# A gated delta-rule attention with two dense blocks: output products over stacked partitions, right-hand sides and kept halves of two tiles joined

## Chip, cores and metric

One core of one Trainium2 chip. The metric is the device time of one execution in microseconds (us); lower is better.

## The reference, cut to what matters

For 4 batches and 8 heads, 768 tokens, head size 48: with k normalised to length one, a 48 x 48 state per head is read by q (the output) and updated by the delta rule. The result (3072 tokens x 384) then goes through two dense blocks.

```python
for t in range(S):
    kt, vt, bt = (k_n[:, :, t], v[:, :, t], beta[:, :, t, None])
    y[:, :, t] = np.einsum('bhd,bhde->bhe', q[:, :, t], state)
    v_old = np.einsum('bhde,bhd->bhe', state, kt)
    state = state + bt[:, :, :, None] * np.einsum('bhd,bhe->bhde', kt, vt - v_old)
# first block:  ((x @ w1) * (x @ w2)) @ w3 @ w_out
# second block: softmax-weighted units, layer norm, @ w_out
```

## The kernel before

**Chunks.** The recurrence is turned into products over chunks of 64 tokens (`C`). A tile holds one chunk of two batches (`bb` = 0 and 1, on partitions 0 to 63 and 64 to 127); two tiles `g` = 0, 1 (the two pairs of batches) go side by side, and a group `n` holds two such pairs `tt` = 0, 1: 6 groups (`NG`) of 4 tiles (`TPG`). Inside a tile every product is made once per head and batch, 16 small matmuls. Each fp32 matmul leaves two records in the trace, so 16 products read x32.

**One pair of tiles, on TensorE** (`group`, function by function): `k_state` (L1334) takes k times state; VectorE's `right_hand` (L1016) makes v minus that; `apply_inverse` (L1351) multiplies by the inverse of a 32 x 32 triangular block, ScalarE's `keep_u` (L1185) keeps the first half of u; `cross_half` (L1363), `right_hand2` (L1025), `apply_inverse` and `keep_u` again give the second half. `outputs` (L1378 and L1380) makes y as two accumulating products per head and batch, q times state (48 rows) and the masked q k^T (`pt`, 64 rows) times u. `add_state` (L1391) adds k^T u to the state that stays in PSUM, and `keep_state` (L1198) copies it to `st`. Then y is transposed (L1406) and split into high and low halves as input of the first dense block.

**One group ahead.** During the pair `tt` = 0 of group n, `grams` (L1322) makes the products k k^T and q k^T of the four tiles of group n + 1, into one pair of PSUM banks: ScalarE copies the diagonal blocks (`keep_diagonal`, L1164) and the corner (`keep_corner`, L1172), VectorE masks the rest into `pt` (`keep_pt`, L894), and only then the next tile's `grams` may start. From the diagonal blocks VectorE solves the triangular systems of group n + 1 (L900 to L1008: `system_rows`, `coefficients`, `substitute`, `eights_*`, `below_*`, `stationary`) in pieces that are put between its other work. POOL turns two small blocks and scales v.

**Fills.** Between these steps TensorE works on the dense block: `fill` puts one unit `up` (L1422, 18 matmuls of 128 x 256) into each of 8 slots of a pair; unit i waits for VectorE's product (L1044) of unit i - 2. In group 0 there is nothing yet to work on, and the slots take parts of w3 times w_out instead (`w3_wout`, L1435, 128 x 384, 64 parts of which 40 run ahead of group 0 and `FILLS` spreads 24). The order on every engine is written out by hand in `group` of `tensor`, `vector`, `scalar` and `sync`. The state of a tile, `kqs`, holds k and q of a head side by side, on partitions 64 * bb to 64 * bb + 47.

**Opening.** SP's and ScalarE's queues load k and q of group 0, then w3 and w_out. TensorE warms up, makes the first four grams, and waits for w_out.

```python
for bb in range(2):
    rk = slice(64 * bb, 64 * bb + D)
    r = slice(64 * bb, 64 * bb + C)
    if q >= NP:
        pe.matmul(chain[g][r, hc(h)], kqs[rk, par, tile, h, C:P], st[rk, g, hc(h)], start=True, stop=False)
    ins = pe.matmul(chain[g][r, hc(h)], pt[r, par, tile, h, :], uu[r, g, hc(h)], start=q < NP, stop=True)
```

## Time and profile before

| what | value |
|---|---|
| median of 3 runs | 785.2 us (782.42 to 785.26) |
| the profiled execution, whole | 785.01 us |
| its span, first to last instruction | 782.9 us |
| mean granted TensorE clock | 0.993 of full |
| TensorE busy | 758.2 us, 97% of the span |
| VectorE, ScalarE, POOL busy | 58%, 44%, 8% |

A line of the timeline is: start in us, duration in us, engine, line, operation, what it writes and reads, how many, and in brackets the idle time before it with what ended it. Instructions on TensorE overlap, so their rate is read from the starts of neighbouring lines and not from their own durations. All times are on the clock of the span.

### The profile page before, as it was taken

How to read it: one execution, taken by the hardware profiler on the slowest of the kernel's cores; microseconds unless marked ns; L12 is line 12 of the kernel's file. 1: busy time of each engine (PE TensorE's matmuls, PEld its weight loads, DVE VectorE, ACT ScalarE, POOL GpSimd, SP SyncE). 2: the span in 40 equal slices, each digit the busy share in tenths (PEclk: the TensorE clock that was granted, in tenths of full speed). 3: DMA queues.
4: the chain of work that ended last, by engine and by line, in shares of the span. 5: the costliest groups of instructions: out<-in, count | busy, mean ns of one | idle time of the engine just before them, and what ended most of it. 6: DMA issues, size and time to landing. Idle time of an engine off the chain costs nothing.

```text
span 782.9 us, 22421 instructions
## 1 busy us (share of the span) xinstructions
PE 758.2 (97%) x9594; PEld 684.0 (87%) x9594; DVE 457.7 (58%) x782; ACT 347.6 (44%) x750; POOL 64.4 (8%) x96
## 2 busy tenths in 40 slices
PE   7999899999999999999999999999999999999997
PEld 6567799989989998998999888888899999999987
DVE  2955945974794598388522354443366656665663
ACT  5745346235434623634234344444344444445443
POOL 1560200100010010001000000000000000000000
PEclk9999999999999999999999999999999999999999
DMA  9940460342035025103101476540000000000001
GB/s 296 396 103 23 106 163 30 70 110 83 30 83 150 30 69 139 54 30 117 42 30 44 155 242 192 159 147 1 1 21 21 22 22 22 23 23 21 21 20 31
DMA packets 37551, 65.38 MB, mean 84 GB/s; under 512 B 3992, under 2 KB 26648, under 8 KB 36504
## 3 DMA queue, kind: packets, MB, share of 16 engines
q1 hardware_dynamic: 34760, 58.48, 25.3%
q10 hardware_dynamic: 2704, 5.60, 2.3%
q8 instruction: 71, 1.16, 0.7%
q14 instruction: 16, 0.13, 0.1%
HBM read 45.19 MB, written 18.87 MB: 82 GB/s over the span
## 4 chain that ended last, share of the span: by engine, by line
PE 84%; DVE 7%; DMA 3%; ACT 2%; issue 2%; SPq 0%; DVEq 0%
PE ps L1422 24%; PE ps L542 13%; PE ps L506 13%; PE ps L519 12%; PE ps L1322 5%; PE ps L1378 3%; DVE tmp L970 3%; PE ps L531 3%; PE ps L1380 3%; PE ps L1334 3%; DMA vs<-in_vtok 2%; PE ps L1435 2%; PE ps L1391 2%; PE ps L1351 1%; DVE rr L1025 1%
## 5 line engine op out<-in xcount | busy, mean ns | idle before, releaser
L1227 ACT COPY asb<-ps 128x256 f32<-128x256 f32 x96 | 35.8, 373 | 154.3 <-PE ps L1422 153.5
L1044 DVE TENSOR_TENSOR msb<-asb,ps 128x256 f32<-128x256 f32 x96 | 39.9, 415 | 87.3 <-ACT asb L1227 82.1
L542 PE MATMUL ps<-woh,uth 128*128 128x384 f32 x192 | 64.7, 337 | 0.5 <-DVE utl L459 0.5
L542 PE MATMUL ps<-woh,utl 128*128 128x384 f32 x192 | 64.5, 336 | 0.0
L542 PE MATMUL ps<-wol,uth 128*128 128x384 f32 x192 | 64.3, 335 | 0.0
L1422 PE MATMUL ps<-xh,w1h 128*128 128x256 f32 x288 | 57.3, 308 | 6.6 <-DVE msb L1044 6.6
L894 DVE TENSOR_TENSOR pt<-ps,mask 128x512 f32<-128x512 f32 x24 | 16.6, 690 | 77.2 <-ACT a L1172 77.2
L459 DVE TENSOR_TENSOR utl<-ps,uth 128x512 fp32r<-128x512 f32 x48 | 31.1, 687 | 47.9 <-ACT uth L349 47.9
L335 ACT ACTIVATE e<-ps,stats 128x1024 f32<-128x1024 f32 x24 | 26.8, 1117 | 67.6 <-DVE stats L425 67.6
L506 PE MATMUL ps<-mh,w34h 128*128 128x512 f32 x144 | 56.0, 389 | 0.0
L506 PE MATMUL ps<-ml,w34h 128*128 128x512 f32 x144 | 56.0, 389 | 0.0
L506 PE MATMUL ps<-mh,w34l 128*128 128x512 f32 x144 | 56.0, 389 | 0.0
L1185 ACT COPY uu<-ps 32x384 f32<-32x384 f32 x96 | 45.2, 471 | 14.4 <-PE ps L1351 13.2
L1422 PE MATMUL ps<-xh,w2h 128*128 128x256 f32 x288 | 50.8, 286 | 0.0
L1422 PE MATMUL ps<-xl,w2h 128*128 128x256 f32 x288 | 50.8, 286 | 0.0
L1422 PEld LDWEIGHTS ps<-xh,w1h 128*128 128x128 f32 x288 | 40.7, 191 | 11.5 <-DVE msb L1044 7.4
L1422 PE MATMUL ps<-xh,w1l 128*128 128x256 f32 x288 | 50.6, 285 | 0.0
L1422 PE MATMUL ps<-xh,w2l 128*128 128x256 f32 x288 | 50.6, 285 | 0.0
L1422 PE MATMUL ps<-xl,w1h 128*128 128x256 f32 x288 | 50.1, 282 | 0.0
L1322 PE MATMUL ps<-kqs 48*64 48x128 f32 x768 | 46.9, 273 | 2.7 <-DVE pt L894 1.2
L1322 PEld LDWEIGHTS ps<-kqs 48*64 48x64 f32 x768 | 42.3, 134 | 7.1 <-issue 6.6
L431 DVE SCALAR_TENSOR_TENSOR mfirst<-ps,e 128x1024 f32<-128x1024 f32 x24 | 29.4, 1225 | 31.8 <-ACT e L335 31.8
(155 smaller groups left out, 1744.5 us busy)
## 6 DMA issues: line engine op xcount, KB each, us to landing
m_dram<-msb SPq DMA_DIRECT2D x42, 256.0 KB, 2.1
mrest<-m_dram SPq DMA_DIRECT2D x36, 256.0 KB, 5.9
kqs<-in_kq SPq DMA_DIRECT2D x20, 384.0 KB, 7.4
vs<-in_vtok SPq DMA_DIRECT2D x6, 768.0 KB, 11.0
ks<-in_ktok SPq DMA_DIRECT2D x5, 768.0 KB, 7.0
mfirst<-m_dram SPq DMA_DIRECT2D x12, 256.0 KB, 5.6
out<-wst SPq DMA_DIRECT2D x12, 192.0 KB
out<-wst SPq DMA_DIRECT2D x48, 48.0 KB, 1.5
```

The source lines that it names most:

```text
L335: act.activation(e[:, :], hb[s], ACT.Exp, bias=nmax[:, s:s + 1], accum_out=es[:, s:s + 1]).then_inc(expd, 1)
L431: dve.scalar_tensor_tensor(out=ubuf[:, s, :], in0=hb[s], scalar=1.0, in1=e[:, :], op0=ALU.mult, op1=ALU.mult, accum_out=us[:, s:s + 1]).th ...
L459: dve.tensor_tensor(utl[:, j, :, :], tb[j].rearrange("p (k c) -> p k c", c=P), uth[:, j, :, :].bitcast(F32), ALU.subtract).then_inc(ut_low, 1)
L506: ins = pe.matmul(hbank[par][k], w[:, f, k * P:(k + 1) * P], mm[:, u, f % UF, :, :].rearrange("p t c -> p (t c)"), start=(f == 0 and j == ...
L519: ins = pe.matmul(hb[slot % 2][:, c * 512:(c + 1) * 512], xx[:, slot, k, :], w[:, k, c * 512:(c + 1) * 512], start=(j == 0 and k == 0), st ...
L531: ins = pe.transpose(tb[j][:, k * P:(k + 1) * P], ubuf[:, s, c:c + P], ident[:, :])
L542: ins = pe.matmul(ob[s], xx[:, j, k, :], w[:, 4 * j + k, :], start=(j == 0 and k == 0 and p == 0), stop=(j == 1 and k == 3 and p == 2))
L1044: dve.tensor_tensor(msb[:, f // 2 % 2, f % 2, :], asb[:, f % 2, :], bbank[f % 2], ALU.mult).then_inc(product, 1)
L1185: ins = act.copy(uu[rows, g, :], chain[g][rows, :])
L1227: act.copy(asb[:, f % 2, :], abank[f % 2]).then_inc(a_kept, 1)
L1322: ins = pe.matmul(gbank[64 * bb:64 * bb + C, h, :], kqs[r, par, tile, h, 0:C], kqs[r, par, tile, h, :], start=True, stop=True)
L1422: ins = pe.matmul(bank, w[:, k, cols], xx[:, par, k, :], start=(j == 0 and k == 0), stop=(j == 2 and k == KD - 1))
```

## The change

The state moves onto the other half of the partitions: of batch `bb` it now stands on partitions 64 * (1 - bb), below or above that batch's u, in one buffer `us`; q stands in `kqs` in the same way beside the masked q k^T, which VectorE now writes into `kqs` as well. So `outputs` makes one product per head and batch over 112 or 128 partitions in place of two. `k_state` and `grams` read rows of the other half than they write. The mask of a tile takes two instructions of 64 partitions. `right_hand` and `right_hand2` take one instruction of 128 x 768 for both tiles, `keep_u` two of 64 x 768. In the opening, k is loaded ahead of q and has its own grams (64 columns), those with q come after three of the w3 products; w_out moves to ScalarE's queue; diagonals are copied ahead of corners; `FILLS` and `WARM` change, and in group 0 the first gram of group 1 follows `apply_inverse`, and `eights_first` and `eights_products` follow `right_hand`.

```diff
-        kqs = buf("kqs", [P, 2, TPG, H, P])
+        kqs = buf("kqs", [P, 2, TPG, 3, H, C])
...
-        pt = buf("pt", [P, 2, TPG, H, C])
...
-        uu = buf("uu", [P, NP, DM])
+        us = buf("us", [P, NP, 2, DM])
         ysb = buf("ysb", [P, NP, DM])
-        st = buf("st", [112, NP, DM])
...
+        both = ps[:, 0:NP, 0:DM]
         gbank = ps[:, 2:4, :].rearrange("p b (h c) -> p (b h) c", c=P)
-        first_gbank = [ps[:, b:b + 2, :].rearrange("p b (h c) -> p (b h) c", c=P) for b in (4, 6, 0, 2)]
+        first_a = [ps[:, b, :].rearrange("p (h c) -> p h c", c=C) for b in (0, 1, 6, 7)]
+        first_p = [ps[:, b, :].rearrange("p (h c) -> p h c", c=C) for b in (2, 3, 6, 7)]
...
-        FILLS = {(0, 0): 3, (0, 1): 3, (0, 2): 3, (0, 3): 3, (0, 4): 3, (0, 5): 3, (0, 6): 2, (0, 7): 2, (1, 0): 2}
+        FILLS = {(0, 0): 6, (0, 1): 4, (0, 2): 3, (0, 3): 3, (0, 4): 2, (0, 5): 2, (0, 6): 1, (0, 7): 1, (1, 0): 2}
         FIRST_W34 = KF - 3
-        WARM = 9
+        WARM = 6
...
+        def state_rows(bb):
+            return slice(64 * (1 - bb), 64 * (1 - bb) + D)
+
+        def loaded_rows(bb):
+            return slice(64 * (1 - bb), 64 * (1 - bb) + (64 if bb else D))
+
+        def u_rows(bb):
+            return slice(64 * bb, 64 * bb + C)
+
+        STACK = (slice(0, 64 + D), slice(0, P))
...
-                    sp.dma_start(kqs[64 * bb:64 * bb + D, n % 2, 2 * tt:2 * tt + 2, :, :],
-                                 kq[n, bb, :, tt]).then_inc(kq_in[n % 2][tt], 16)
+                    r = loaded_rows(bb)
+                    for part in range(2):
+                        sp.dma_start(kqs[r, n % 2, 2 * tt:2 * tt + 2, part * (1 + bb), :, :],
+                                     kq[n, bb, 0:r.stop - r.start, tt, :, part]).then_inc(kq_in[n % 2][tt], 16)
...
-            for tile in range(TPG):
-                sp.dma_start(kqs[0:D, 0, tile:tile + 1, :, :],
-                             kq[0, 0, :, tile // 2, tile % 2:tile % 2 + 1]).then_inc(kq_first[tile], 16)
+            def load_first(part, tt, arrived):
+                sp.dma_start(kqs[loaded_rows(0), 0, 2 * tt:2 * tt + 2, part, :, :],
+                             kq[0, 0, 0:D, tt, :, part]).then_inc(arrived[tt], 16)
+
+            for tt in range(2):
+                load_first(0, tt, k_first)
             load_w3(0)
-            sp.dma_start(wos[0], wo1[:, 0:4, :]).then_inc(wo1_in[0], 16)
             load_w3(1)
+            for tt in range(2):
+                load_first(1, tt, q_first)
+            load_w3(2)
             load_v(0)
-            for f in range(2, 5):
-                load_w3(f)
-            for j in range(2 * KF):
+            load_w3(3)
+            for j in range(KF):
                 load_w(j)
+            load_w3(4)
+            sp.wait_ge(w34_done, 2)
+            load_kq(1, 0)
             load_w3(5)
-            load_k(1)
+            for j in range(KF, 2 * KF):
+                load_w(j)
+            sp.wait_ge(w34_done, 4)
+            load_kq(1, 1)
             for f in range(6, KF):
                 load_w3(f)
-            sp.wait_ge(w34_done, 2)
-            load_kq(1, 0)
-            sp.wait_ge(w34_done, 4)
-            load_kq(1, 1)
+            load_k(1)
             sp.wait_ge(w34_done, KF)
             load_v(1)
             for n in range(1, NG):
...
+            const(pool.memset(us[HB:C, :, 1, :], 0.0))
...
-            def keep_pt(n, par, tile, gbank=gbank):
-                i = TPG * n + tile
-                dve.wait_ge(gram_kept, i + 1)
-                dve.tensor_tensor(pt[:, par, tile, :, :], gbank[:, :, C:P],
-                                  mask[:, tile % NP, :].unsqueeze(1).to_broadcast([P, H, C]), ALU.mult).then_inc(pt_made, 1)
+            def masked(par, tile, bank):
+                for bb in range(2):
+                    r = u_rows(bb)
+                    ins = dve.tensor_tensor(kqs[r, par, tile, 1 + bb, :, :], bank[r],
+                                            mask[r, tile % NP, :].unsqueeze(1).to_broadcast([C, H, C]), ALU.mult)
+                ins.then_inc(pt_made, 1)
+
+            def keep_first_pt(tile):
+                dve.wait_ge(p_gram, tile + 1)
+                masked(0, tile, first_p[tile])
+
+            def keep_pt(n, par, tile):
+                dve.wait_ge(gram_kept, TPG * n + tile + 1)
+                masked(par, tile, gbank[:, :, C:P])
...
-            def right_hand(n, par, tt, g):
-                q = TPG * n + NP * tt + g
-                dve.wait_ge(ks_done, q + 1 - NP)
-                dve.wait_ge(v_scaled, n + 1)
-                tile = NP * tt + g
-                dve.tensor_tensor(rr[:, g, :], vs[:, par, tile * DM:(tile + 1) * DM], chain[g],
-                                  ALU.subtract).then_inc(rhs, 1)
-
-            def right_hand2(n, tt, g):
-                q = TPG * n + NP * tt + g
-                dve.wait_ge(cross, q + 1)
-                for bb in range(2):
-                    rows = half_rows(bb, g, 1)
-                    before = vs[rows, 0, g * DM:(g + 1) * DM] if q < NP else rr[rows, g, :]
-                    ins = dve.tensor_tensor(rr[rows, g, :], before, chain[g][rows, :], ALU.subtract)
-                ins.then_inc(rhs2, 1)
+            def of_both(par, tt):
+                return vs[:, par, NP * tt * DM:NP * (tt + 1) * DM].rearrange("p (g n) -> p g n", n=DM)
+
+            def right_hand(n, par, tt):
+                dve.wait_ge(ks_done, TPG * n + NP * tt)
+                if n == 0:
+                    dve.wait_ge(v_first, 2)
+                else:
+                    dve.wait_ge(v_scaled, n)
+                dve.tensor_tensor(rr[:, :, :], of_both(par, tt), both, ALU.subtract).then_inc(rhs, NP)
+
+            def right_hand2(n, tt):
+
+                q = TPG * n + NP * tt
+                dve.wait_ge(cross, q + NP)
+                given = of_both(0, 0) if q < NP else rr[:, :, :]
+                dve.tensor_tensor(rr[:, :, :], given, both, ALU.subtract).then_inc(rhs2, NP)
...
-                    right_hand(n, par, 0, 0)
-                    right_hand(n, par, 0, 1)
+                    right_hand(n, par, 0)
                 product_of(0, 0)
...
+                right_hand(n, par, 1)
+                if n == 0:
+                    eights_first(n + 1)
+                    eights_products(n + 1)
...
-            dve.wait_ge(consts, 11)
-            for tile in range(3):
-                keep_pt(0, 0, tile, first_gbank[tile])
+            dve.wait_ge(consts, 12)
             system_rows(0)
...
-            keep_pt(0, 0, 3, first_gbank[3])
+            for tile in range(TPG):
+                keep_first_pt(tile)
...
-            def keep_u(q, g, half, done, kept):
-                act.wait_ge(done, q + 1)
+            def keep_u(q, half, done, kept):
+
+                act.wait_ge(done, q + NP)
                 if q == 0 and half == 0:
                     act.wait_ge(w_low, 2 * NP)
-                for bb in range(2):
-                    rows = half_rows(bb, g, half)
-                    ins = act.copy(uu[rows, g, :], chain[g][rows, :])
-                ins.then_inc(kept, 1)
+                    for g in range(NP):
+                        for bb in range(2):
+                            rows = half_rows(bb, g, half)
+                            ins = act.copy(us[rows, g, bb, :], chain[g][rows, :])
+                else:
+                    for bb in range(2):
+                        ins = act.copy(us[u_rows(bb), :, bb, :], both[u_rows(bb)])
+                ins.then_inc(kept, NP)
...
-                    rows = slice(64 * bb, 64 * bb + D)
-                    ins = act.copy(st[rows, g, :], sbank[g][rows, :])
+                    rows = state_rows(bb)
+                    ins = act.copy(us[rows, g, bb, :], sbank[g][rows, :])
...
                     a_of(0)
-                    if early:
+                    if early and n > 0:
                         keep_gram(n + 1, 0)
-                    keep_u(q, 0, 0, u1_done, u1_kept)
-                    keep_u(q + 1, 1, 0, u1_done, u1_kept)
+                    keep_u(q, 0, u1_done, u1_kept)
+                    if early and n == 0:
+                        keep_gram(n + 1, 0)
...
+            def load_first(part, tt, arrived):
+                act.dma_start(kqs[loaded_rows(1), 0, 2 * tt:2 * tt + 2, 2 * part, :, :],
+                              kq[0, 1, :, tt, :, part]).then_inc(arrived[tt], 16)
+
+            for tt in range(2):
+                load_first(0, tt, k_first)
+            act.dma_start(wos[0], wo1[:, 0:4, :]).then_inc(wo1_in[0], 16)
             act.dma_start(bet[:, :, :], beta).then_inc(beta_in, 16)
             act.dma_start(wos[1], wo1[:, 4:8, :]).then_inc(wo1_in[1], 16)
+            for tt in range(2):
+                load_first(1, tt, q_first)
             act.dma_start(ks[:, 0, :], ktok[0]).then_inc(k_in[0], 16)
             act.preload_act_table(ACT.Sqrt)
-            keep_gram(0, 0, first_gbank[0])
-            keep_gram(0, 1, first_gbank[1])
-            keep_gram(0, 2, first_gbank[2])
-            keep_gram(0, 3, first_gbank[3])
+            for tile in range(TPG):
+                keep_diagonal(0, tile, first_a[tile])
+            keep_corner(0, 0, first_a[0])
+            keep_corner(0, 1, first_a[1])
             roots(0)
-            scale_first_v()
-            for f in range(FIRST_W34):
-                for j in range(4 * f - 4, min(4 * f, 2 * KF)):
-                    if j >= 0:
-                        high_w(j)
+            keep_corner(0, 2, first_a[2])
+            keep_corner(0, 3, first_a[3])
+            for f in range(2):
+                keep_w34(f)
+                scale_first_v(f)
+            for f in range(2, FIRST_W34):
+                for j in range(4 * (f - 2), min(4 * (f - 1), KF)):
+                    high_w(j)
...
+            def first_grams(part, tile, bank, done):
+                for h in range(H):
+                    for bb in range(2):
+                        r = state_rows(bb)
+                        ins = pe.matmul(bank[u_rows(bb), h, :], kqs[r, 0, tile, 0, h, :],
+                                        kqs[r, 0, tile, part * (1 + bb), h, :], start=True, stop=True)
+                ins.then_inc(done, 1)
...
-                        r = slice(64 * bb, 64 * bb + D)
-                        ins = pe.matmul(gbank[64 * bb:64 * bb + C, h, :], kqs[r, par, tile, h, 0:C],
-                                        kqs[r, par, tile, h, :], start=True, stop=True)
+                        r = state_rows(bb)
+                        ins = pe.matmul(gbank[u_rows(bb), h, :], kqs[r, par, tile, 0, h, :],
+                                        kqs[r, par, tile, 0:2 + bb:1 + bb, h, :], start=True, stop=True)
...
-                        rk = slice(64 * bb, 64 * bb + D)
-                        r = slice(64 * bb, 64 * bb + C)
-                        if q >= NP:
-                            pe.matmul(chain[g][r, hc(h)], kqs[rk, par, tile, h, C:P], st[rk, g, hc(h)],
-                                      start=True, stop=False)
-                        ins = pe.matmul(chain[g][r, hc(h)], pt[r, par, tile, h, :], uu[r, g, hc(h)],
-                                        start=q < NP, stop=True)
+                        r = STACK[bb] if q >= NP else u_rows(bb)
+                        ins = pe.matmul(chain[g][u_rows(bb), hc(h)], kqs[r, par, tile, 1 + bb, h, :],
+                                        us[r, g, bb, hc(h)], start=True, stop=True)
                 ins.then_inc(y_done, 1)
...
-                    if early:
+                    if early and n > 0:
                         grams(n + 1, 0)
                     if tt == 0:
                         pe.wait_ge(inverse, n + 1)
                     apply_inverse(n, par, tt, 0, rhs, u1_done)
+                    if early and n == 0:
+                        grams(n + 1, 0)
...
-                grams(0, tile, first_gbank[tile])
-            pe.wait_ge(gram_kept, 1)
-            pe.wait_ge(pt_made, 1)
+                pe.wait_ge(k_first[tile // 2], 32)
+                first_grams(0, tile, first_a[tile], gram)
             for half in range(2):
                 for f in range(2):
                     w3_wout(f, range(KF // 2 * half, KF // 2 * (half + 1)))
             for f in range(2, FIRST_W34):
                 w3_wout(f, range(KF))
-            pe.wait_ge(gram_kept, 3)
-            pe.wait_ge(pt_made, 3)
+                if f == 2:
+                    for tile in range(TPG):
+                        pe.wait_ge(q_first[tile // 2], 32)
+                        if tile >= 2:
+                            pe.wait_ge(gram_kept, tile + 1)
+                        first_grams(1, tile, first_p[tile], p_gram)
+            pe.wait_ge(gram_kept, TPG)
...
-        return split(a).transpose(3, 1, 7, 4, 0, 2, 5, 6)
+        return split(a).transpose(3, 1, 7, 4, 0, 2, 5, 6).reshape(NG, 2, D, 2, NP, H * C)
...
-        "kq": np.stack([columns(k), columns(q)], axis=6).reshape(NG, 2, D, 2, NP, H, P),
+        "kq": np.pad(np.stack([columns(k), columns(q)], axis=5), [(0, 0), (0, 0), (0, 64 - D)] + [(0, 0)] * 4),
```

How the rows stand on TensorE at the outputs of the second pair of group 0 (a row of `order` is line, operation, out<-in, shape, count; `xh`, `xl`, `w2l` belong to `up`). Before:

```order
L1422 MATMUL ps<-xh,w2h 128x256 x3
L1422 MATMUL ps<-xl,w2h 128x256 x3
L1422 MATMUL ps<-xh,w2l 128x256 x3
L1378 MATMUL ps<-st,kqs 64x48
L1380 MATMUL ps<-uu,pt 64x48
...
L1391 MATMUL ps<-uu,ks 48x48 x16
```

After the change:

```order
L1472 MATMUL ps<-xh,w2l 128x256 x3
L1430 MATMUL ps<-us,kqs 64x48 x16
L1441 MATMUL ps<-us,ks 48x48 x16
L1430 MATMUL ps<-us,kqs 64x48 x16
L1441 MATMUL ps<-us,ks 48x48 x16
L1472 MATMUL ps<-xh,w1h 128x256 x3
```

The alternating rows of L1378 and L1380, 16 of each a tile, have become 16 of L1430.

On VectorE, from the first pair of group 1 on (L1044 is the product of a unit, L900 the start of the next solve). Before:

```order
L1016 TENSOR_TENSOR rr<-vs,ps 128x384 x2
L1044 TENSOR_TENSOR msb<-asb,ps 128x256
L894 TENSOR_TENSOR pt<-ps,mask 128x512
L1044 TENSOR_TENSOR msb<-asb,ps 128x256
L894 TENSOR_TENSOR pt<-ps,mask 128x512
L1025 TENSOR_TENSOR rr<-rr,ps 32x384 x4
```

After:

```order
L1053 TENSOR_TENSOR rr<-vs,ps 128x768
L1078 TENSOR_TENSOR msb<-asb,ps 128x256
L918 TENSOR_TENSOR kqs<-ps,mask 64x512 x2
L1078 TENSOR_TENSOR msb<-asb,ps 128x256
L918 TENSOR_TENSOR kqs<-ps,mask 64x512 x2
L1060 TENSOR_TENSOR rr<-rr,ps 128x768
```

The right-hand sides have shrunk from 2 and 4 instructions to 1 each, the mask has grown from 1 to 2.

On TensorE's opening after the change (L1360 are the first grams, k's above and q's below; before, 64 products of 64x128 stood in the first place and none in the second):

```order
L1540 MATMUL ps<-ident 128x128 x6
L1360 MATMUL ps<-kqs 64x64 x64
L1485 MATMUL ps<-vs,kqs 128x384 x8
L1485 MATMUL ps<-mfirst,kqs 128x384 x8
L1485 MATMUL ps<-vs,kqs 128x384 x4
L1485 MATMUL ps<-mfirst,kqs 128x384 x4
L1360 MATMUL ps<-kqs 64x64 x64
```

The products with q have moved behind the first 24 parts of w3 times w_out.

## Rows read from the trace of the kernel before

**Rows 1.** The page: share of the chain that ended last.
```profile
PE 84%; DVE 7%; DMA 3%; ACT 2%; issue 2%; SPq 0%; DVEq 0%
```

**Rows 2.** Timeline, TensorE, outputs of the second pair of group 2.
```profile
229.94 0.52 PE L1422 MATMUL ps<-xh,w2l 128*128 128x256 f32 x3
230.39 0.33 PE L1378 MATMUL ps<-st,kqs 48*64 48x48 f32 x4
...
232.29 0.92 PE L1391 MATMUL ps<-uu,ks 64*48 64x48 f32 x32
233.01 0.32 PE L1378 MATMUL ps<-st,kqs 48*64 48x48 f32 x4
...
234.88 0.92 PE L1391 MATMUL ps<-uu,ks 64*48 64x48 f32 x32
```

**Rows 3.** Timeline, TensorE, outputs of the first pair, which has no state.
```profile
67.58 1.14 PE L1380 MATMUL ps<-uu,pt 64*64 64x48 f32 x32
68.55 0.89 PE L1391 MATMUL ps<-uu,ks 64*48 64x48 f32 x32
```

**Rows 4.** Chain of waits: start, us, what.
```profile
29.97 17.65 PE ps L1435 x54
...
159.45 3.50 PE ps L1422 x18
168.67 2.35 PE ps L1422 x18
```

**Rows 5.** Timeline, TensorE, transposes between two units.
```profile
207.83 0.82 PE L1406 MATMUL ps<-ident,ysb 128*128 128x128 f32 x6
208.40 0.60 PE L1422 MATMUL ps<-xh,w1h 128*128 128x256 f32 x3
```

**Rows 6.** Timeline, one turn of the gram banks: TensorE, ScalarE, VectorE.
```profile
247.39 1.96 PE L1322 MATMUL ps<-kqs 48*64 48x128 f32 x32
...
252.64 1.96 PE L1322 MATMUL ps<-kqs 48*64 48x128 f32 x32
...
249.40 1.49 ACT L1164 COPY gd<-ps 32x256 f32<-32x256 f32 x4 [1.53 <-PE ps L1322]
250.91 0.74 ACT L1172 COPY a<-ps 32x256 f32<-32x256 f32 x2
...
251.68 0.69 DVE L894 TENSOR_TENSOR pt<-ps,mask 128x512 f32<-128x512 f32 x1 [3.36 <-ACT a L1172]
```

**Rows 7.** Timeline, last gram of a group to the last third of its second pair.
```profile
196.00 1.96 PE L1322 MATMUL ps<-kqs 48*64 48x128 f32 x32
217.23 0.88 PE L1351 MATMUL ps<-rr,ti 32*32 32x48 f32 x64
228.05 0.62 PE L1422 MATMUL ps<-xh,w1h 128*128 128x256 f32 x3 [0.16 <-DVE msb L1044]
...
214.37 1.18 DVE L1016 TENSOR_TENSOR rr<-vs,ps 128x384 f32<-128x384 f32 x2
...
222.97 2.26 DVE L1025 TENSOR_TENSOR rr<-rr,ps 32x384 f32<-32x384 f32 x4
```

**Rows 8.** Costliest groups: a VectorE subtraction of 128 x 768.
```profile
L218 DVE TENSOR_TENSOR w34l<-h,w34h 128x768 fp32r<-128x768 f32 x3 | 2.9, 959 | 1.1 <-ACT w34h L210 1.1
```

**Rows 9.** Opening: a DMA issue (line, count, KB, us to landing) and the timeline.
```profile
vs<-in_wo SPq DMA_DIRECT2D x1, 768.0 KB, 13.8
...
17.07 7.05 PE L1435 MATMUL ps<-vs,kqs 128*128 128x384 f32 x16 [3.57 <-DMA vs<-in_wo]
...
63.55 1.96 PE L1322 MATMUL ps<-kqs 48*64 48x128 f32 x32 [0.33 <-DVE pt L894]
...
82.65 0.88 PE L1351 MATMUL ps<-rr,ti 32*32 32x48 f32 x64 [2.71 <-DVE rr L1016]
...
16.67 1.93 DVE L900 STREAM_TRANSPOSE amat<-gd 128x1024 f32<-128x1024 f32 x1 [0.82 <-ACT gd L1164]
...
44.93 2.10 DVE L1008 STREAM_TRANSPOSE ti<-xt 128x1024 f32<-128x1024 f32 x1
```

63 lines of the change are left out of this document (29 added, 34 removed).

## The prediction

> **What bounds it now.** The chain of waits comes first: TensorE is 84% of what ended last, VectorE 7% [rows 1]. So a microsecond of TensorE's work is a microsecond of the kernel, except where TensorE stands and waits for VectorE. The timeline of the attention part then shows three things. One: the outputs of a tile take 230.39 to 232.29 and 233.01 to 234.88, 1.90 and 1.87 us for 64 records [rows 2]. Two: the grams turn in a ring. A gram starts at 247.39, the next at 252.64, 5.25 us later, and between them lie its own 1.96, ScalarE's copies to 251.65, and VectorE's mask from 251.68 to 252.37 [rows 6]: each begins when the one before ends, so the ring sets the pace and TensorE's other work of that turn fits inside it. Three: in the second pair TensorE is ready for a unit at about 226.5 and starts it at 228.05, after VectorE [rows 7].
>
> **How fast a product of 48 columns can go.** Full-array fp32 products of 384 columns run at 17.65 / 54 = 327 ns a record [rows 4], so 0.85 ns a column and 41 ns for 48 columns. The masked products alone (64 rows, 64 weight columns, 48 moving columns, `bb` alternating) need 0.97 us for 32 records, 30 ns each [rows 3], and the pair of products 1.87 / 64 = 29 ns [rows 2]. That is under 41, so the two halves of the array, with different rows and different columns, work at once. The state update has 48 weight columns and takes 0.72 / 32 = 22.5 ns [rows 2]: the rate goes with the weight columns, 0.45 ns each, so loading sets it.
>
> **Term 1, the outputs.** 22 of 24 tiles (all but the first pair) drop from 64 records to 32. The unknown is a record's price. The two products of a head now use all the rows and only differ in columns; no row of this trace has that. Bounds: 29 ns if they still overlap; 41 ns and a few for the start, 43 to 51, if they stream one after the other; 41 plus a load of 64 columns at 0.45, 70 ns, if the load is not hidden either; and 95 ns, the step of the 128-column transposes, (208.40 - 207.83) / 6 [rows 5], as the far end. I take 29, since its row is the same stationary and moving size on the same engine and only the row group differs. Then a tile saves 0.94 us, a pair 1.87. Against that, outputs and state update no longer share an array shape. Going from a unit to the products costs 0.09 us (229.94 + 3 x 0.12 = 230.30, start at 230.39) [rows 2]; three more such changes a pair cost 0.27. Net 1.6 us a pair.
>
> **Term 2, the ring.** The mask becomes two instructions of 64 partitions with the same 512 elements each. A VectorE instruction's time goes with elements per partition (384 take 0.57 to 0.59 in a row of four or two [rows 7], 512 take 0.69 alone [rows 6], of which some 0.07 overlaps the next), so the second adds about 0.62. It lies in the ring: three turns in each of five groups, 9.3 us if nothing gives. This is a real loss that the change brings with it: after 247.39 the last gram comes 17.6 us later in place of 15.7. k_state, the state update and the grams reading one half and writing the other keep their sizes: nothing.
>
> **Term 3, the right-hand sides.** `right_hand` becomes one instruction of 768: 0.96 [rows 8] for 1.18; `right_hand2` one of 0.96 for 2.26 [rows 7], 1.3 less. From the last gram (196.00) to VectorE's right-hand side (215.55) are 19.5 us of nearly unbroken VectorE work, and TensorE reaches its use at 217.23, 1.7 later [rows 7]. Now VectorE needs 19.5 + 0.6 - 0.2 = 19.9, TensorE 21.2 - 1.6 = 19.6: VectorE is just ahead as the bound, and takes back 0.5 of the first pair's gain. From there to 228.05 the old way is 12.5; minus 1.3 for `right_hand2` and minus 1.0 that VectorE idled for ScalarE's copy of a unit (which is now long there) gives 10.2. Last gram to that unit: 32.05 before, 30.2 now, 1.85 less.
>
> **Groups 1 to 4**: +1.87 (ring) - 1.85 - 1.6 (outputs of the second pair) = -1.6 each, -6.4. In group 1 the wait was followed by a unit of 3.50 us in place of 2.35 [rows 4], which no other group shows; I put it down to the clock falling in the wait, and with a shorter wait it should go: -1.2. **Group 5** has no ring and no solve: 2 x 1.6 = -3.2. ScalarE's `keep_u` loses a little; it was hidden behind the units and stays hidden. Doubled DMA issues of k and q are on SP's queue, which has microseconds between them.
>
> **Opening and group 0.** TensorE waited until 17.07 for w_out, issued at 3.12 and landed 13.8 later behind 4 x 192 KB of k and q and 512 KB of w3 on one of two queues [rows 9]: 2048 KB in some 15 us, 137 KB/us a queue. Now it follows 512 KB on the other queue: 1280 KB, so near 11. The 46 parts ahead of the inverse take 46 x 0.65 = 29.9, the four grams of q 4.2, waits 0.7: 45.8. VectorE's solve began at 16.67 and its last step ended at 47.0 [rows 9]. The k grams are half as wide and the 16 diagonal copies (4 x 1.5 us) come first: start near 13.3, end 43.6. So the inverse is applied near 46, but the four masks of group 0 (2 x 0.65 each) now stand behind the solve, to 48.8, and the second gram of group 1 waits for them and for its own: 52.3. With two turns of 5.86 the last gram starts at 64.0, against 63.55 [rows 9]. Then 4 us of solve steps have moved behind the right-hand side, which TensorE had waited 2.71 for [rows 9]: it comes 3.0 earlier, and the moved 4 us delay the later part of that pair by about as much. With its outputs, group 0 ends 0.5 to 2.5 earlier; I take -1.2.
>
> **Sum**: -1.2 - 6.4 - 1.2 - 3.2 = -12.0 on the profiled 785.0, so 773.0. The median of the runs is 0.2 above the profiled one, which changes nothing. A change of 0.5% (about 4 us) is what a measurement of this kernel can tell from none.
>
> **Rivals.**
> *The columns stream in turn.* Two products that use the same rows might share what feeds the rows, so they go one after the other at 43 to 51 ns, 47 in the middle. For it: nothing in the trace shows overlap with common rows. Against it: nothing but likeness. A tile then takes 1.50 and saves 0.37; a pair nets 0.5 in place of 1.6, over 11 pairs 12 us less gain, of which VectorE's bound in four first pairs returns 2 to 3. Result 773 + 9.5 = 782.
> *The weights are not hidden* (the other side). `bb` alternates row groups now, and the load for one half can run while the other multiplies; with all rows in use by both there is no other half. Price 70 ns, 2.2 us a tile: 0.35 slower than before, and 0.27 for the shapes, about +1.0 a pair against -1.6. Over 11 pairs 28 us worse than my sum; the first pairs of groups 1 to 4 get back 0.5 each, and waits for VectorE shrink by some 4 more: 773 + 22 = 795. It decides from about 47 to 49 ns a record on, where the sum passes zero. Against it: full-array records show a load of 128 columns hidden behind a stream at 327 ns for 384 columns, so a load of the same rows can be hidden, though there the stream is long.
> The Trainium skill (TensorE: Matmul & The Clock Gate, Part 3, the mechanism) says that a weight load overlaps matmuls in flight only when the row group differs. By that rule the change would come out at this rival; the full-array rows speak against taking it literally, and the page itself excepts the background weight buffer. The Trainium skill (TensorEngine Tiling, key properties) says on the other side that tiles of 128 x 64 are two and load and multiply independently, which is my forecast; no run here shows it yet.
> *The opening does not come earlier.* If both queues share the bandwidth otherwise and TensorE starts near 14 to 17, its extra 6 us ahead of the inverse (grams of q, 3 more parts) show: group 0 ends 4 to 7 later, 773 + 6 = 779.
>
> **Chances and range.** Forecast 0.58 (767 to 778, nearly all over 0.5% faster, 0.56 and 0.02); late opening 0.10 (0.07 faster, 0.03 same); columns in turn 0.18, 778 to 787 (0.06 faster, 0.11 same, 0.01 slower); weights not hidden 0.14, 787 to 820, slower. Faster 0.69, same 0.16, slower 0.15. The range takes the first three: 766 to 787.
>
> **What would show it.** Right: 32 records of L1430 start within 0.93 to 1.0 us a tile, with `add_state` rows unchanged at 0.72 and gaps near 0.1 around them; the grams of a group 5.8 to 5.9 apart; the wait before the unit after the second `apply_inverse` under 0.8 us; TensorE's first w3 product near 11. A step of 1.4 to 1.6 us a tile is the first rival, 2.2 or more the second. The forecast is wrong in its base if the ring still turns in 5.25, or if the masks' two halves overlap.

## The result and the profile after

The changed kernel takes 773.6 us (median of 4 runs, 771.74 to 774.38) against 785.05 us (4 runs, 782.42 to 785.26), a ratio of 0.9858 with a 95% interval of 0.9831 to 0.9886: 11.45 us faster, where 12.0 were forecast. The profiled execution has a span of 772.7 us, 10.2 less than the one before. Of the page after, the share of the chain that ended last, and three groups of instructions (busy us, mean ns, idle us before them and what ended it):

```profile
PE 80%; DVE 9%; ACT 6%; issue 4%; DMA 2%; DVEq 0%
...
L918 DVE TENSOR_TENSOR kqs<-ps,mask 64x512 f32<-64x512 f32 x48 | 33.0, 687 | 73.3 <-ACT a L1204 72.8
...
L1472 PE MATMUL ps<-xh,w1h 128*128 128x256 f32 x288 | 57.4, 308 | 6.2 <-DVE msb L1078 6.2
...
L1376 PE MATMUL ps<-kqs 48*64 48x128 f32 x640 | 39.3, 272 | 13.3 <-DVE kqs L918 13.3
```

TensorE is less of the chain than in [rows 1], VectorE and ScalarE more. The last line is the ring: TensorE now waits 13.3 us for masks of 687 ns each. Timeline after, TensorE, from the second `apply_inverse` of the second pair of group 2 over its outputs (they answer to [rows 2] and [rows 7]):

```profile
226.23 0.88 PE L1405 MATMUL ps<-rr,ti 32*32 32x48 f32 x64
227.05 0.63 PE L1472 MATMUL ps<-xh,w1h 128*128 128x256 f32 x3
...
229.39 1.14 PE L1430 MATMUL ps<-us,kqs 112*64 112x48 f32 x32
230.46 0.92 PE L1441 MATMUL ps<-us,ks 64*48 64x48 f32 x32
231.31 1.14 PE L1430 MATMUL ps<-us,kqs 112*64 112x48 f32 x32
232.38 0.92 PE L1441 MATMUL ps<-us,ks 64*48 64x48 f32 x32
233.23 0.62 PE L1472 MATMUL ps<-xh,w1h 128*128 128x256 f32 x3
```

A tile's outputs take 1.07 us from start to start, 33.4 ns a record, in place of 1.90. The unit after `apply_inverse` starts without the wait that [rows 7] has. One turn of the ring after, answering to [rows 6]:

```profile
244.88 1.97 PE L1376 MATMUL ps<-kqs 48*64 48x128 f32 x32
246.89 1.49 ACT L1196 COPY gd<-ps 32x256 f32<-32x256 f32 x4 [1.53 <-PE ps L1376]
248.40 0.74 ACT L1204 COPY a<-ps 32x256 f32<-32x256 f32 x2
249.17 1.39 DVE L918 TENSOR_TENSOR kqs<-ps,mask 64x512 f32<-64x512 f32 x2 [3.36 <-ACT a L1204]
...
250.82 1.96 PE L1376 MATMUL ps<-kqs 48*64 48x128 f32 x32 [0.82 <-DVE kqs L918]
```

5.94 us in place of 5.25: the mask's two halves do not overlap, and the difference is the second one. The opening and group 0 after, answering to [rows 9]:

```profile
6.91 7.09 PE L1360 MATMUL ps<-kqs 48*64 48x64 f32 x128 [2.24 <-DMA kqs<-in_kq]
13.94 1.01 PE L1485 MATMUL ps<-vs,kqs 128*128 128x384 f32 x1
...
49.56 0.88 PE L1405 MATMUL ps<-vs,ti 32*32 32x48 f32 x64
50.37 1.96 PE L1376 MATMUL ps<-kqs 48*64 48x128 f32 x32
...
68.23 1.96 PE L1376 MATMUL ps<-kqs 48*64 48x128 f32 x32 [1.02 <-DVE kqs L918]
...
15.65 1.93 DVE L933 STREAM_TRANSPOSE amat<-gd 128x1024 f32<-128x1024 f32 x1 [15.65 <-ACT gd L1196]
```

Here the last gram is 4.7 us later than before, not 0.5. Where the time went, by marks that both traces have (us from start to start; the grams of a group are those that it makes for the next):

| stretch | before | after | difference | forecast |
|---|---|---|---|---|
| start to the first gram in group 1 | 111.28 | 113.64 | +2.4 | -1.2 |
| to the first gram in group 2 | 68.98 | 65.51 | -3.5 | -2.8 |
| to that in group 3 | 67.13 | 65.73 | -1.4 | -1.6 |
| to that in group 4 | 67.13 | 65.53 | -1.6 | -1.6 |
| to group 5's first `apply_inverse` | 67.14 | 65.94 | -1.2 | -1.6 |
| to the first L506, the next stage | 75.80 | 70.88 | -4.9 | -3.2 |
| to the end of the span | 325.44 | 325.47 | 0.0 | 0 |

The sum of the differences is the span's, -10.2. About 1.5 us of the -4.9 in the last stretch but one was not forecast: before, TensorE waits 1.79 us for VectorE ahead of the last six units, and 0.8 us after it has gone on its records slow down. Over the 4 us shown the mean is 0.58, and from 444 to 447 it is 0.50, the 1.2 GHz level. The kernel before at this place: the wait, three records at the low clock (0.84 us where the others take 0.52), the busy time in 4 us (us and count of PE, PEld, DVE, ACT, POOL, then the granted clock), and the chain of waits before and after:

```profile
442.92 0.62 PE L1422 MATMUL ps<-xh,w1h 128*128 128x256 f32 x3 [1.79 <-DVE msb L1044]
...
444.44 0.84 PE L1422 MATMUL ps<-xh,w2h 128*128 128x256 f32 x3
```

```profile
443.00:447.00 4.00, 4.00 (x22) 4.00 (x23) 2.20 (x3) 0.41 (x2) 0.00 (x0) 0.58 0.17 66
```
```profile
442.92 14.70 PE ps L1422 x108
```
```profile
434.17 13.22 PE ps L1472 x108
```

The wait after is 1.36 us, and the clock stays at 1.00. The slow unit of group 1 in the kernel before [rows 4] looks the same: TensorE waits 1.80 us for VectorE until 159.45, and the granted clock is 0.50 from 161 to 163. A third such stretch of the kernel before is its opening: after the wait for w_out until 17.07 the mean granted clock is 0.60 from 18 to 21. The kernel after has none of the three. The mean clock of its four runs is 0.999 to 1.000, against 0.992 to 0.996 in the 11 runs of before that stand beside the first experiments.

### The profile page after: what moved, and what is told of

It is laid out like the page before. It is cut to its first block, busy times and chain, and to the rows that moved or that the text cites. A ratio compares the mean times of both kernels' runs of the same rounds, so it can differ in the third digit from the quotient of the medians.

```text
span 772.7 us, 21207 instructions
## 1 busy us (share of the span) xinstructions
PE 741.6 (96%) x9012; PEld 664.5 (86%) x9012; DVE 451.2 (58%) x759; ACT 339.5 (44%) x704; POOL 66.6 (9%) x97
## 4 chain that ended last, share of the span: by engine, by line
PE 80%; DVE 9%; ACT 6%; issue 4%; DMA 2%; DVEq 0%
PE ps L1472 19%; PE ps L542 13%; PE ps L506 13%; PE ps L519 12%; PE ps L1376 5%; PE ps L1485 4%; ACT gd L1196 3%; PE ps L1388 3%; PE ps L531 3%; DVE kqs L918 2%; PE ps L1430 2%; ACT a L1204 2%; PE ps L1441 2%; PE ps L1360 1%; PE ps L1405 1%
## 5 line engine op out<-in xcount | busy, mean ns | idle before, releaser
L918 DVE TENSOR_TENSOR kqs<-ps,mask 64x512 f32<-64x512 f32 x48 | 33.0, 687 | 73.3 <-ACT a L1204 72.8
L506 PE MATMUL ps<-mh,w34h 128*128 128x512 f32 x144 | 56.0, 389 | 0.0
L506 PE MATMUL ps<-ml,w34h 128*128 128x512 f32 x144 | 56.0, 389 | 0.0
L506 PE MATMUL ps<-mh,w34l 128*128 128x512 f32 x144 | 56.0, 389 | 0.0
L1376 PE MATMUL ps<-kqs 48*64 48x128 f32 x640 | 39.3, 272 | 13.3 <-DVE kqs L918 13.3
L1196 ACT COPY gd<-ps 32x256 f32<-32x256 f32 x96 | 34.8, 363 | 35.2 <-PE ps L1376 32.2
L1376 PEld LDWEIGHTS ps<-kqs 48*64 48x64 f32 x640 | 34.9, 133 | 17.0 <-issue 16.4
## 6 DMA issues: line engine op xcount, KB each, us to landing
vs<-in_vtok SPq DMA_DIRECT2D x6, 768.0 KB, 10.2
```

What stands on the lines that cost most here:

```text
L506: ins = pe.matmul(hbank[par][k], w[:, f, k * P:(k + 1) * P], mm[:, u, f % UF, :, :].rearrange("p t c -> p (t c)"), start=(f == 0 and j == ...
L918: ins = dve.tensor_tensor(kqs[r, par, tile, 1 + bb, :, :], bank[r], mask[r, tile % NP, :].unsqueeze(1).to_broadcast([C, H, C]), ALU.mult)
L1196: ins = act.copy(gd[rows, tile * H:(tile + 1) * H, :], gbank[rows, :, HB * half:HB * (half + 1)])
L1376: ins = pe.matmul(gbank[u_rows(bb), h, :], kqs[r, par, tile, 0, h, :], kqs[r, par, tile, 0:2 + bb:1 + bb, h, :], start=True, stop=True)
```

## The experiments

**Whose alternation makes the products overlap.** After, with the loops of `outputs` exchanged, so that 8 products for one column half follow each other.

```diff
-                for h in range(H):
-                    for bb in range(2):
+                for bb in range(2):
+                    for h in range(H):
```

> The change with one edit: in the outputs all 8 products of one batch (112 rows, columns 0 to 63) come first, then all 8 of the other (128 rows, columns 64 to 127), in place of by turns. Theory (products on common rows but different columns overlap when they alternate): nothing is left to overlap, a record goes from 33 ns to 41 ns (48 columns at 0.85) and more, 45 to 60, so a tile goes from 1.07 us to 1.45 to 1.9 and the kernel gains 7 to 15 us on 773.6: 781 to 789. Rival (they never overlap and the rate is set by the weight load alone): a record stays at 33 ns and the time at 773 to 775.

Measured: 786.07 us, 1.0035 of before (1.0018 to 1.0051). Timeline of its TensorE:

```profile
231.80 1.87 PE L1430 MATMUL ps<-us,kqs 112*64 112x48 f32 x32
233.60 0.92 PE L1441 MATMUL ps<-us,ks 64*48 64x48 f32 x32
```

The same 32 records need 1.80 us, 56 ns each against 33.4. So the overlap comes from alternating between the two column halves, and without it the whole gain is gone (+12.5 us).

**The price of a product, by doubling it.** After, each stacked product issued twice in a row.

```diff
-                        ins = pe.matmul(chain[g][u_rows(bb), hc(h)], ...
+                        for again in range(2 if q >= NP else 1):
+                            ins = pe.matmul(chain[g][u_rows(bb), hc(h)], ...
```

> The change with each stacked output product issued twice in a row (the second overwrites the first). Theory (TensorE is the bound and a stacked record costs 33 ns): 32 records more in 22 tiles at 33 ns are 1.07 us a tile, 23.5 us, of which the first pairs of groups 1 to 4 give back up to 1 us each because VectorE is ahead there: +19 to +24, 793 to 797. If the same column half twice in a row cannot overlap, a record costs 41 ns or more and the sum is +30 or more. Rival (the outputs are hidden): under +10.

Measured: 794.45 us, 1.0133 (1.0103 to 1.0162), +20.8 against after.

```profile
207.59 2.11 PE L1431 MATMUL ps<-us,kqs 112*64 112x48 f32 x64
209.62 0.92 PE L1442 MATMUL ps<-us,ks 64*48 64x48 f32 x32
```

64 records take 2.03 us, 31.7 ns each; the 32 added ones take 0.96 us a tile, 30 ns each, and 20.8 us over 22 tiles give the same 30. So two neighbours may share a column half as long as the next two take the other. Undoing the stacking itself, two accumulating products in the new layout, was not tried.

**The right-hand sides alone.** Before, with `right_hand` and `right_hand2` joined as in the change.

```diff
-                right_hand2(n, 1, 0)
-                right_hand2(n, 1, 1)
+                right_hand2(n, 1)
...
+                dve.tensor_tensor(rr[:, :, :], given, both, ALU.subtract).then_inc(rhs2, NP)
```

> The kernel before with only the right-hand sides joined (one instruction of 128x768 for both tiles, twice a pair); outputs, masks, copies and opening as before. Theory: right_hand2 ends 1.3 us earlier, the wait of TensorE ahead of the unit after the second apply_inverse (1.4 to 1.9 us in groups 1 to 4) shrinks by 1.3, and the slow unit in group 1 goes: -5 to -7 us, 778 to 780. Rival (VectorE is late there for the contended subtraction and not for right_hand2, or the clock fell for another reason): -2 us or less, 783 to 785.

Measured: 777.47 us, 0.9927 (0.9902 to 0.9952), -7.0 against the 784.49 of before measured with it. So 7 us are to be had with the outputs left as they were, about as much as the split mask costs in the next run. Not all of it is shorter waiting: the granted clock stays at 1.00 both in group 1 and in the last six units, which is worth some 1.2 and 1.5 us.

```profile
436.10 13.21 PE ps L1417 x108
```

Ahead of these six units TensorE waits 1.86 us, longer than the 1.79 of the kernel before, and still they run at full speed. So the length of the wait does not by itself decide whether the clock falls.

**The split mask alone.** Before, with the mask in two instructions of 64 partitions.

```diff
+                for bb in range(2):
+                    r = slice(64 * bb, 64 * bb + C)
+                    ins = dve.tensor_tensor(pt[r, par, tile, :, :], gbank[r, :, C:P], ...
```

> The kernel before with only the mask in two instructions of 64 partitions instead of one of 128. Theory (the mask lies in the ring of grams, copies and mask): each of 15 turns goes from 5.25 us to 5.87, +9.3 us, and VectorE's later work adds up to 0.6 in groups 1 to 4, so 794 to 797. Rival (two halves of the partitions overlap on VectorE, or the ring has slack): within 2 us of 785.

Measured: 791.13 us, 1.0097 (1.0059 to 1.0136): +6.6, less than expected, though the ring turns in 5.94 as expected (grams at 184.57 and 190.52). From the first gram for a group to that for the next it has 252.26 to 319.96, 67.70 us, only 0.57 over before, and from the last gram (270.10) to that mark 49.86 where before has 263.12 to 314.52, 51.40. Something gives back 1.5 us behind the ring. VectorE and POOL at that place, first before, then with the split mask:

```profile
217.49 2.78 POOL L856 TENSOR_TENSOR vs<-vs,nrm 128x1536 f32<-128x1536 f32 x1
218.08 3.28 DVE L970 TENSOR_TENSOR tmp<-amat,xt 128x1024 f32<-128x1024 f32 x1
```
```profile
224.48 1.22 DVE L973 TENSOR_TENSOR tmp<-amat,xt 128x1024 f32<-128x1024 f32 x1
224.56 3.76 POOL L856 TENSOR_TENSOR vs<-vs,nrm 128x1536 f32<-128x1536 f32 x1
```

Before, POOL's scaling of v starts first and VectorE's product of the solve, started 0.59 us later, takes 3.28 us; with the split mask VectorE is 0.08 ahead and takes 1.22, and POOL pays with 3.76 in place of 2.78. The next experiment tests this.

**POOL's scaling out of VectorE's way.** Before, with one wait more.

```diff
                 pool.wait_ge(coef, GCOEF * (n + 1))
+                pool.wait_ge(solve, GSOLVE * n + MERGED8 + 1)
```

> The kernel before with one more wait in POOL's scaling of v (L856): it starts only when VectorE's first wide product of the solve (L970, 128 x 1024) is done. Nothing is left out. In the traces so far L970 takes 3.28 us where POOL's scaling starts 0.59 us ahead of it (217.49 and 218.08, before) and 3.72 us where it starts 0.12 ahead (joined_rhs_alone), but 1.22 us where it starts 0.08 behind (split_mask_alone, batch_outer) and 1.65 in the kernel after (219.27 and 218.74); POOL's own instruction takes 2.78 us when first and 3.75 to 3.79 when second. Theory (the one that starts second pays, and VectorE is what TensorE waits for in the second pair of each group of before): L970 at 1.22, 2.06 us less in each of groups 1 to 4; TensorE's wait there of 1.5 us goes, and one that costs a slow clock behind it in group 1 and ahead of the last six units; last Gram product of a group to the first of the next 51.40 -> 49.8 (that of split_mask_alone is 49.86); in all 777 to 779, so -6 to -8. Rival (VectorE's product is long for a reason of its own, or the collision moves on to L979 or L1025 behind it): L970 or the next instruction longer by 2 us, total 784.7 within 1.5.

Measured: 777.93 us, 0.9921 (0.9898 to 0.9945), -6.7 against 784.6.

```profile
215.85 2.77 POOL L857 TENSOR_TENSOR vs<-vs,nrm 128x1536 f32<-128x1536 f32 x1 [2.03 <-DVE tmp L971]
...
214.36 1.22 DVE L971 TENSOR_TENSOR tmp<-amat,xt 128x1024 f32<-128x1024 f32 x1
215.61 1.22 DVE L980 TENSOR_REDUCE gd<-tmp 128x128 f32<-128x1024 f32 x1
```

The product takes 1.22, the reduction beside POOL's scaling is not stretched, and from the last gram to the next group's first are 49.87 us (257.88 to 307.75). One added wait brings more than half of what the whole change brings. It and the joined right-hand sides shorten the same wait of TensorE; both together were not run on the kernel before, and need not add up.

**The mask released by bank.** After, tiles 0 to 2 masked in four instructions of 64 x 256, heads 0 to 3 first; the next grams of heads 0 to 3 start when their PSUM bank is free.

```diff
+                for part in range(2):
+                    hs = slice(H // 2 * part, H // 2 * (part + 1))
+                    for bb in range(2):
...
+                    ins.then_inc(pt_made if part else pt_low, 1)
```

> The change with the mask of the first three tiles of a group split by PSUM bank as well (four instructions of 64 x 256, heads 0 to 3 of both batches first), and the next grams of heads 0 to 3 released after the first bank, those of heads 4 to 7 after the second. Theory (the mask is in the ring, 5.94 us a turn): the first two instructions take about 0.8 us in place of 1.3 and the second bank's mask runs under the first 8 products, so a turn goes to 5.3 to 5.5 and 15 turns give 6.5 to 9.5 us; VectorE pays 0.3 us more a tile, hidden: 764 to 768. Rival (the next thing behind the ring, ScalarE's copies or VectorE's products, takes it over): 771 to 774.

Measured: 765.82 us, 0.977 (0.9737 to 0.9804), -7.8 against after.

```profile
185.76 1.96 PE L1393 MATMUL ps<-kqs 48*64 48x128 f32 x32 [0.28 <-DVE kqs L936]
...
190.04 1.75 DVE L936 TENSOR_TENSOR kqs<-ps,mask 64x256 f32<-64x256 f32 x4 [2.34 <-ACT a L1215]
191.16 1.96 PE L1393 MATMUL ps<-kqs 48*64 48x128 f32 x32 [0.28 <-DVE kqs L936]
```

The mask itself grew to 1.75 us, but TensorE starts before it ends: 5.40 us a turn, 0.54 less, 15 turns, 8.1 us. The ring's time is the kernel's.

**Outputs of both tiles in one go**, then the state of both.

```diff
                     outputs(n, par, tt, 0)
-                    add_state(n, par, tt, 0)
                     outputs(n, par, tt, 1)
+                    add_state(n, par, tt, 0)
```

> The change with both tiles' outputs first and both state updates after them, so two changes of array shape fewer a pair (unit, out, out, add, add, unit). Theory (a change of shape costs about 0.13 us: add_state takes 0.85 from start to start where it took 0.72): 11 pairs x 0.26 = -2.9, 770 to 772. Rival (the surplus is in the records themselves, or the later keep_state delays k_state): 773 to 775, with 32 records still at 1.07.

Measured: 770.98 us, 0.9836 (0.9799 to 0.9873), -2.6 against after, less than the scatter of four runs can settle by itself (the two intervals overlap). The trace settles it:

```profile
227.95 2.07 PE L1430 MATMUL ps<-us,kqs 112*64 112x48 f32 x64
...
231.53 0.62 PE L1472 MATMUL ps<-xh,w1h 128*128 128x256 f32 x3
```

A pair takes 3.58 us (227.95 to 231.53) in place of 3.84, with two changes between the two kinds of product fewer: each costs about 0.13 us, and 11 pairs give 2.9.

**Both of these**, the mask released by bank and the outputs together, in one kernel.

> bank_gate and outputs_together in one kernel. If their gains are on TensorE's path and independent they add: 761 to 766. If one hides the other, no better than the better of the two.

Measured: 764.29 us, 0.9753 (0.9721 to 0.9785): 20.4 us under before and 9.3 under the change, where the two gains alone add up to 10.4.

**The state's half left out.** After, with products over the 64 rows of u alone: q times state is not computed.

```diff
-                        r = STACK[bb] if q >= NP else u_rows(bb)
+                        r = u_rows(bb)
```

> The change with the state half left out of the outputs: only the 64 rows of masked q k^T times u, one product per head and batch in the 64x64 shape (the q times state part of y is not computed). Theory (a stacked record costs no more than a 64-row one, and the shape changes cost the rest): 32 records take 0.93 us as in the first pair, add_state 0.72, so a pair loses 4 x 0.13: 11 x 0.54 = -6, 767 to 769. Rival (the 112 to 128 rows themselves cost): outputs fall to 0.93 while add_state stays at 0.85.

Measured: 768.79 us, 0.981 (0.9778 to 0.9843), -4.8 against after, with runs from 765.88 to 772.37. Its TensorE:

```profile
225.66 0.96 PE L1430 MATMUL ps<-us,kqs 64*64 64x48 f32 x26
226.41 0.25 PE L1441 MATMUL ps<-us,ks 64*48 64x48 f32 x2
...
228.60 0.62 PE L1472 MATMUL ps<-xh,w1h 128*128 128x256 f32 x3
```

29 ns a record as in [rows 3], and records of the state update stand between those of the outputs: a pair takes 2.94 us (225.66 to 228.60), 0.90 less than after and less than the 3.3 that was expected. So the gain is not one of cheaper records alone: part of it is that the two kinds of product mix, which they do not with full rows. Of the 0.90 us only the second pair's counts: from 175.61 to 240.25, 64.64 us a group against 65.6. In the first pair the gain is lost again: from the last gram to the second pair's outputs are 32.23 us in both kernels (193.43 to 225.66, and 197.16 to 229.39). VectorE is the bound there, as the forecast had it.

**The opening's clock.** After, with 11 opening products in place of 6.

> The kernel after with 11 opening products of the identity in place of 6, so that TensorE doesn't wait 2.24 us for the first k before the first Gram products. Nothing is left out. In the kernel after those products take 1.7 us a tile (7.09 us for four) and four copies of ScalarE follow at this pace, so that VectorE's system starts at 15.65. Theory (the opening is paced by the slow k products): with no wait ahead of them the products run at up to twice the rate, about 1.0 us a tile, ScalarE's copies (1.49 us each) become the bound, the system starts at 13.8 to 14.6, the w_out product starts when its first weights have landed, about 12.6 instead of 13.9, the first inverse is applied at 48.3 instead of 49.6; total 772.4 (771.5 to 773.5), so -1.2 against the kernel after. Rival (TensorE's 36 us of products in the opening are paced by their data and by each other, and the clock of the first Gram products is not set by the wait): products of 1.7 us a tile as now, first inverse at 49.6, total 773.6, no change.

Measured: 773.23 us, 0.988 (0.9829 to 0.993), no difference from after that can be told.

```profile
6.73 2.17 PE L1360 MATMUL ps<-kqs 48*64 48x64 f32 x64
9.31 2.08 PE L1360 MATMUL ps<-kqs 48*64 48x64 f32 x64 [0.40 <-DMA kqs<-in_kq]
12.76 5.40 PE L1485 MATMUL ps<-vs,kqs 128*128 128x384 f32 x16 [1.36 <-DMA vs<-in_wo]
```

The k grams do run at 34 ns a record in place of 55, and the inverse is applied at 47.68 in place of 49.56; the span is 1.1 shorter (771.6), inside the scatter of runs. Now TensorE waits for w_out until 12.76, so 11 was never to be had. The expectation put the slow grams down to the wait ahead of them; the next run speaks against that.

**The old shares of the w_out product.** After, with the old `FILLS`.

> The kernel after with the pieces of the w_out product shared out over group 0's positions as in the kernel before (3, 3, 3, 3, 3, 3, 2, 2 in the first pair in place of 6, 4, 3, 3, 2, 2, 1, 1). Nothing is left out. Theory (in group 0 TensorE waits 1.25, 1.02 and 1.02 us for VectorE's masks between the four Gram products, and pieces ahead of a Gram product stand in those waits, pieces behind the last one do not): four pieces move behind the last Gram product, each 0.36 us a weight tile and two or three of these a piece, so the end of group 0 comes 1 to 3 us later and the total is 774.6 to 776.6. Rival (behind the last Gram product TensorE waits 0.65, 0.81 and 0.34 us for ScalarE and VectorE, which take up what moves there): 773.6, within 0.5.

Measured: 772.62 us, 0.9849 (0.9818 to 0.988): the rival, nothing lost. The new shares bring nothing.

```profile
5.47 7.19 PE L1360 MATMUL ps<-kqs 48*64 48x64 f32 x128 [0.80 <-DMA kqs<-in_kq]
```

Here k came at 5.47 rather than 6.91. TensorE waited 0.80 us for it in place of 2.24, and the grams took 56 ns a record all the same, so the length of that wait is not what slows them. The inverse was applied at 45.52; three shares fewer ahead of it explain 2.0 of the 4.0 us. The rest is scatter: in `batch_outer`, `outputs_doubled`, `outputs_together`, `half_rows` and `bank_gate`, which open just as the kernel after does, the inverse is applied at 46.87 to 48.75, and 49.56 in the kernel after is the latest of all.

**The fastest kernel with the longer opening.**

> The fastest kernel so far (mask released bank by bank, outputs of both tiles in one go, state added for both behind; 764.3) with 11 opening products in place of 6. Nothing is left out. If the wait for the first k costs what the theory on it says, 763.1 (762 to 764.3); by its rival 764.3. Either way the gains of the two earlier edits should stand.

Measured: 763.38 us, 0.9747 (0.9708 to 0.9786), 0.9 under `both_of_these`, which 4 runs each cannot tell from none.

## Why the forecast held, step by step

- **Outputs (term 1): right.** 29 ns a record were taken, 33.4 measured; the changes of shape were put at 0.27 a pair, and beside the dearer record 0.13 shows (the first state update, 0.85 for 0.72). A pair fell from 5.34 to 3.84, 1.50 against 1.6. The rival with columns in turn (43 to 51) and the one with weights not hidden (70) would have shown 1.4 to 2.2 us a tile against the 1.07 measured. `batch_outer` shows how near they were: 56 ns if only the order of the loops is another, past the forecast's own break-even of 47 to 49, and that kernel is indeed 0.35% slower than before. By the rule that the Trainium skill (TensorE: Matmul & The Clock Gate, Part 3) gives, that a weight load overlaps only matmuls of another row group, the two orders should be equally slow, since all these products use rows of every group; the runs disagree, 33.4 against 56 ns. What the Trainium skill (TensorEngine Tiling, key properties) says of column tiles that load and multiply independently agrees with them.
- **The ring (term 2): right in mechanism, a little small.** 5.87 a turn were forecast, 5.94 to 6.14 measured; from first to last gram 18.0 in group 2 where 17.6 were said.
- **Right-hand sides (term 3): right in size, incomplete in cause.** Last gram to unit took 29.89 (197.16 to 227.05) where 30.2 were said and 32.05 was before. VectorE's two instructions are 0.95 each, as [rows 8] promised. But L970's 3.28 us stood in the old trace beside the POOL row that stretched it, and the forecast took VectorE's work there as fixed. After, VectorE starts 0.53 ahead of that POOL instruction and needs 1.65. VectorE's last product before that unit ends at 225.50, 1.55 us early, so in the changed kernel this gift of 1.6 lies in slack (worked out from these rows, not run).
- **Slow clock: half seen.** The unit of 3.50 us in group 1 is gone (group 1 gave 3.5, forecast 2.8). That the last six units lose as much in the same way (14.70 for 13.22) was not seen, and gave 1.5 more. Nor is the mechanism settled: the forecast expected the clock to stay up because the wait is shorter, but in `joined_rhs_alone` it stays up behind a longer one (1.86 us). The low clock is in nearly every run of the kernel before (mean 0.993) and hardly shows in the four after (0.999 to 1.000); what decides it stays open.
- **Opening and group 0: wrong.** +2.4 us in place of -1.2. The step that failed is the start of the w_out product "near 11": its first weights, landed 10.3 us after their issue at 2.26, are there at 12.6, and the k grams held TensorE until 13.94, as k came 2.24 us after the warm-up's end and the grams then took 55 ns a record. Of the 3.6 us by which the inverse is late (49.56 for 46) this is 2.9; the last gram comes at 68.23 for 64.0. The rival "the opening does not come earlier" was right as to the opening, and too dear: behind the last gram 2.3 of the 4.7 us come back (63.55 to 111.28 before, 68.23 to 113.64 after), 1.5 of it from the outputs. The moved solve steps bring little: TensorE's wait of 2.71 us is down to 0.34, but waits of 1.55 and 0.92 us for VectorE follow in the same pair. The 46 was missed in every execution with this opening (46.87 at the best), but part of the +2.4 is the profiled execution's own bad luck. And the inverse is no earlier than before (49.56 for 49.72) although the w_out product starts 3.1 us earlier and the low clock of the old opening is gone: the grams of q and three more shares now stand ahead of it. An estimate of what the rebuilt opening does: `joined_rhs_alone`, with the old one, has its first gram of group 1 at 110.03; three longer turns add 2.1 and the outputs of one pair take off 1.5, so 110.6. With the new opening it is 113.64 (after), 111.76 (`warm_eleven`) and 111.54 (`old_fills`), 0.9 to 3.0 later. So the new opening is more likely a loss than a gain; the old one was not put back by itself.

Group 0 came 3.6 us worse than forecast and the rest 1.8 better, 1.5 of it by a slow clock in the last six units that the forecast had not seen. The second error hid half of the first: 1.8 us off in the profiled execution (10.2 for 12.0), 0.6 in the medians. That the total is so close is in part luck; the terms for the outputs and the ring are right without it, that for the right-hand sides at least in its size.

## What to carry to other kernels

Small products that take all the rows of the array can still run side by side if neighbours in the program write different column halves: try that order of the loops first; here it decides between 33.4 and 56 ns a record. In a ring of two engines on one buffer, release the buffer in pieces, in the order in which the next user takes them; an instruction split that costs time in itself can pay. And before a slow instruction is taken as a fixed price, look at what POOL runs beside it and which of the two started first.

## What was not expected of the hardware

- A VectorE product of two SBUF operands and POOL's scaling of v do not run together: the one that starts second waits for the other's end. Before, POOL ends at 220.27 and VectorE's product at 221.36, 1.09 later; in `joined_rhs_alone` POOL ends at 216.51 and the product, started at 213.86, at 217.58. The other way round, with the split mask, VectorE ends at 225.70 and POOL at 228.32, 2.62 later. VectorE alone needs 1.22, POOL 2.77. VectorE's 1.65 in the kernel after is the same with a shorter POOL copy ahead of it (L892, 0.64). A reduction (1.22) and a subtraction with one operand in PSUM (0.95) beside the same POOL instruction kept their times. The Trainium skill (SBUF — State Buffer, SBUF: two separate sides) states this lock, that the first holds it for its whole instruction and the second fully blocks; the runs agree, and the forecast had passed over it.
- Going between products of 112 x 64 and 64 x 48 costs about 0.13 us.
- Waits of TensorE of 1.79 and 1.80 us were each followed, some 0.8 us after it had gone on, by about 3 us of slow records with the granted clock down to 0.50; behind one of 1.36 us (after) and one of 1.86 (`joined_rhs_alone`) it stayed at 1.00. So these rows give no rule by the length of the wait.
- In the opening the k grams ran at 55 ns a record behind 6 products of the identity and a wait of 2.24 us, at 56 ns behind 6 and a wait of 0.80, and at 34 ns behind 11 and no wait; the same 128 records with q take 3.87 us, 30 ns each, at 31.30. So the grams are quicker where the warm-up is longer, and the length of the wait makes no difference. The granted clock reads 1.00 in all of them; what slowed the grams stays open.
